# Second mixture of experts: TensorE waits for half of an expert's weights first, and for the rest at the second layer

## What is computed

```python
def _moe2_ref(x, w_skip, w_gate, w1, w2):
    do_compute = x @ w_skip > 0
    out = x.copy()
    xc = x[do_compute]
    e_idx = np.argmax(xc @ w_gate, axis=1)        # one expert for a token
    ...                                           # gate_w: its softmax weight
    for e in range(E):
        mask = e_idx == e
        h = np.maximum(xc[mask] @ w1[e], 0.0)     # w1[e]: 512 x 1024
        y[mask] = gate_w[mask, None] * (h @ w2[e])    # w2[e]: 1024 x 512
    out[do_compute] = xc + y
    return out
```

## Time and profile before

| | us |
|---|---|
| three timed runs | 730.63, 733.49, 738.72 |
| their median | 733.49 |
| the profiled execution, its own time | 731.53 |
| its span, first to last instruction | 729.7 |
| PE busy in the span | 652.2 (89%) |
| PE's mean granted clock, as a share of full speed | 0.952 |
| second mixture: first product of its experts | 526.3 |
| second mixture: last scatter issued | 719.6 |

### The profile page before, as it was taken

The page is one execution under the profiler, slowest core; times in us unless marked ns, Lnnn a source line. Parts: engine busy times, 40 slices in busy tenths (PEclk is TensorE's granted clock), DMA queues, the critical chain, the costliest instruction groups (busy, mean ns, idle before and its releaser), DMA issues.

```text
span 729.7 us, 13727 instructions
## 1 busy us (share of the span) xinstructions
PE 652.2 (89%) x4168; PEld 575.2 (79%) x4168; DVE 379.0 (52%) x761; ACT 292.8 (40%) x503; POOL 204.7 (28%) x227
## 2 busy tenths in 40 slices
PE   5697883799999999999999999999599979999793
PEld 4576763489999999999999999876487768777682
DVE  2676687535363545454453636403565476745721
ACT  2365662034352434443432435214155455645520
POOL 1538670220232405060413324030112222222220
PEclk9899997599999999999999999999799999999997
DMA  9999996126182727456371927167175587556221
GB/s 196 203 232 235 269 301 198 37 60 230 49 234 71 213 79 166 158 113 212 72 252 48 251 72 220 58 141 242 24 245 151 156 288 236 161 161 232 42 42 16
DMA packets 94866, 116.14 MB, mean 159 GB/s; under 512 B 55940, under 2 KB 56068, under 8 KB 94800
## 3 DMA queue, kind: packets, MB, share of 16 engines
q1 hardware_dynamic: 77264, 90.83, 41.9%
q0 software_dynamic: 10464, 23.81, 15.9%
q10 hardware_dynamic: 7072, 0.70, 0.7%
HBM read 100.01 MB, written 20.18 MB: 165 GB/s over the span
## 4 chain that ended last, share of the span: by engine, by line
PE 71%; SPq 8%; DMA 6%; DVE 6%; issue 5%; ACT 1%; POOL 1%; POOLq 0%; DVEq 0%; ACTq 0%
PE bank L788 20%; PE bank L794 20%; PE bank L893 15%; SPq L499 5%; DMA xg<-x_moe,ix_take 2%; PE bank L777 2%; SPq L514 2%; DMA out<-y_sb,ix_put 2%; PE bank L766 2%; PE bank L645 2%; PE bank L695 1%; PE bank L717 1%; PE bank L909 1%; DVE col_val L1580 1%; PE bank L678 1%
## 5 line engine op out<-in xcount | busy, mean ns | idle before, releaser
L1454 DVE TENSOR_TENSOR w_lo<-stage,w_hi x120 | 141.6, 1221 | 21.7 <-ACT w_hi L1018 19.5
L1018 ACT CAST w_hi<-stage x120 | 119.6, 1047 | 9.8 <-PEq L935 9.7
L788 PE MATMUL bank<-tok_hi,w_hi 128*128 128x416 f32 x256 | 91.3, 357 | 1.8 <-DVE tok_lo L1636 1.8
L794 PE MATMUL bank<-unit_hi,w_hi 128*128 128x416 f32 x256 | 92.5, 361 | 0.0
L788 PE MATMUL bank<-tok_hi,w_lo 128*128 128x416 f32 x256 | 90.5, 354 | 0.0
L794 PE MATMUL bank<-unit_lo,w_hi 128*128 128x416 f32 x256 | 90.2, 352 | 0.0
L794 PE MATMUL bank<-unit_hi,w_lo 128*128 128x416 f32 x256 | 89.6, 350 | 0.0
L1670 DVE SCALAR_TENSOR_TENSOR unit_lo<-bank,unit_hi 128x416 fp32r<-128x416 f32 x64 | 37.8, 591 | 98.2 <-ACT unit_hi L1104 98.2
L1104 ACT ACTIVATE unit_hi<-bank 128x416 fp32r<-128x416 f32 x64 | 33.2, 519 | 130.7 <-PE bank L788 130.7
L1304 POOL DMA_INDIRECT x_moe<-rows_out,ix_put x32 | 58.7, 1835 | 53.2 <-DVE rows_out L1659 45.9
L788 PE MATMUL bank<-tok_lo,w_hi 128*128 128x416 f32 x256 | 58.7, 350 | 0.0
(11 more groups left out here) (162 smaller groups left out, 1106.1 us busy)
## 6 DMA issues: line engine op xcount, KB each, us to landing
stage<-in_moe_w SPq DMA_DIRECT2D x128, 512.0 KB, 5.6
v_win<-in_v SPq DMA_DIRECT2D x24, 192.0 KB, 6.8
x_moe<-rows_out SPq DMA_DIRECT2D x12, 260.0 KB, 3.3
x_att<-x_sb POOLq DMA_DIRECT2D x12, 256.0 KB, 5.2
x_sb<-x_moe SPq DMA_DIRECT2D x12, 256.0 KB, 2.8
out<-x_moe SPq DMA_DIRECT2D x4, 768.0 KB, 8.6
late_raw<-in_v SPq DMA_DIRECT2D x6, 384.0 KB, 6.9
stage<-in_k SPq DMA_DIRECT2D x6, 256.0 KB, 6.7
```

The source lines that it names most:

```text
L788: last = eng.matmul(ps_unit[f % 2][:, 0:W], w, x, start=(i == 0), stop=(i == len(mine) - 1))
L794: last = eng.matmul(ps_out[chunk][:, 0:W], w[:, WC // 2 + f, chunk * P:(chunk + 1) * P], h[:, f % UNITS, :], start=(f == 0 and i == 0), st ...
L1018: eng.copy(piece(w_hi[n % SETS], j), stage[:, j, :]).then_inc(s_hi, 1)
L1454: eng.tensor_tensor(piece(w_lo[n % SETS], j), stage[:, j, :], piece(w_hi[n % SETS], j).bitcast(F32), ALU.subtract)\
```

## The change

PE's wait ahead of an expert's slots asks for `PIECES * n - 4` pieces, which are the expert's first four, the whole of `w1`. A new wait for all of the expert's pieces stands in each slot, between the first and the second layer. Nothing else differs.

```diff
                 for e in range(E):
                     n = m * E + e
                     hi, lo = w_hi[n % SETS], w_lo[n % SETS]
-                    eng.wait_ge(s_lo, PIECES * n)
+                    eng.wait_ge(s_lo, PIECES * n - PIECES // 2)
                     eng.reg_mov(done, 0)
                     with eng.While(lambda: eng.snap(done) < eng.snap(counts[e])):
@@
                         turn_h(0)
                         products(ps_h[1], up[1], T // 2, T).then_inc(S["h"], 1)
                         eng.wait_ge(S["hth"], sv * 2 + 1)
+                        eng.wait_ge(s_lo, PIECES * n)
                         eng.wait_ge(S["ye"], sv + 1)
                         products(ps_y, down, 0, T // 2)
```

## The result

The change makes the kernel faster by a little: 728.8 us against 733.9 us, medians of 20 runs each, with a ratio of 0.9929 and a 95% interval of 0.9906 to 0.9951. That is 5.2 us less (3.6 to 6.9). The ratio, and the 5.2 us worked out from it, leave out the few runs in a slower state. Forecast was a ratio of 730.0 / 733.5 = 0.995, 3.5 us less, which lies just outside the small end of that interval.

A forecast was written before the change was run, and what follows sets the result against it. POOL's serial DMA chain was taken to bind, 13.7 us per slot against PE's 13.0, hidden by two weight waits. `y_sb` at 714.3 instead of 717.84 gave 3.5 us less: 728.0 profiled, 730.0 us median; range 724.5 to 735.0.

The forecast's parts named there:

- the sum: Last slot's `y_sb` written at 714.3 instead of 717.84, 3.5 us less; profiled execution 728.0, median forecast 730.0 us.
- The end: Last slot: `y_sb` waits for scatter 12, landing at 714.06, and no longer for PE; written at 714.3.
- The waits and the clock: Before slots 5 and 12: PE starts 3.25 and 3.46 us earlier, and the low clock's 1.53 and 1.28 go too.
- The new wait at nothing: At the second layer, 14 times: passes with 3.4 us in hand, taken as no cost; upper end 1.4 us.
- DVE late in slot 5: PE waits 0.8 us for `ht_lo` in slot 5, leaving PE 4.0 us earlier after it.
- The gather at slot 9: At the turning of slot 9's rows, PE waits up to 3.7 us for POOL's gather; 4.0 us gain becomes 0.1.
- rival B: Earlier weight loads fall on more of POOL's gathers and scatters: 13 us on its chain, less 3.5, 743 us; chance 0.12.
- the mark of a wrong forecast: The forecast is wrong if POOL's steps between 589.99 and 646.42 shift by more than a microsecond.
- The size: Whole kernel: 3.5 us less, forecast 730.0 against 733.49 us, 0.5% less.
- Rival A: POOL keeps up and PE's whole gain comes through: 8.7 us, 724.8 us; chance 0.13.
- the argument against it: Against 743 us: an expert's 4 MB take some 13 us, a whole POOL round, and already meet one gather and scatter.

The follow-up runs named there:

- POOL relieved: The change with POOL's gather and scatter overlapped (ratio 0.9852), or with the last six experts' weight loads cut to an eighth (0.9867), both against the kernel before.
- slot 5 only: Kernel before, with the first wait asking for four pieces at the fourth expert only (slots 5 and 6): ratio 0.9963, 2.7 us less.
- Slot 12 alone: Kernel before, with the first wait asking for four pieces at the last expert only (slots 12 and 13): ratio 0.9958, 3.1 us less.
- the light loads: Last six experts' weight loads cut to 64 of each 512 columns: ratio 0.9986 on the kernel before, 0.9867 on the changed kernel.
- overlap, slot 5 only: Kernel before, with POOL's gather and scatter in flight together and four pieces asked for at the fourth expert only: ratio 0.9908, 6.8 us less.

## Why the prediction was right, and where not

The mechanism was right: both waits fall away, PE gains about 9.5 us of its own (9.7 and 8.8 with POOL relieved), and POOL's chain of one DMA at a time takes back a good part of it. The size agrees with the sum partly by luck, as said under *The end*. Point by point:

- *The waits and the clock.* Right, with 0.56 to 0.6 us left at each change of expert and a clock of 1.00.
- *The new wait at nothing.* Right, as far as one execution with nine of them tells.
- *DVE late in slot 5.* Of the forecast 0.8 us PE's row shows 0.2 in the changed kernel and 0.8 with slot 5 only.
- *The end.* Right: `y_sb` waits for scatter 12, forecast to land 714.06 - 526.27 = 187.8 us into the mixture, and it landed at 717.71 - 529.56 = 188.1. That these agree is luck in part. Scatter 3, ahead of the first removed wait, was issued 0.6 us later into the mixture than in the profile before. From there to scatter 7 POOL gained 1.6 us, where 0.1 was forecast. From scatter 7 to scatter 12 it lost 0.6 us (63.59 before, 64.15 after), where a gain of 0.64 was forecast; 1.0 of it is scatter 10, which took 5.9 us and not 4.9. Slot 12 alone gave 3.1 us, near the 3.4 that the sum leaves to it.
- *The gather at slot 9.* **This is the step that failed**: "PE waits up to 3.7 us there", and "4.0 us of gain have become 0.1". PE was held up along the way instead: 1.1 and 0.4 us at the second layers of slots 6 and 8, where `y_sb` was late because scatters 4 and 6 landed late. At slot 9's rows only 0.2 us were left, at slot 7's 0.3. The 0.8 us for slot 5's rows stand ahead of the first removed wait, and the second profile of the kernel before has them too. Of the 4.0 us, 1.1 were left at slot 9's rows, turned 118.0 us into the mixture and not 119.1 (2.1 in the second profile of the changed kernel, 116.9). I had kept the duration of each of POOL's DMAs as the trace before had it. But DVE's last five splits in slot 5 come earlier (from 76.6 us of the mixture on, before from 80.2), so the loads do, and by the GB/s above their burst moved from the gathers of slots 7 and 9 to the scatters of slots 4 and 6. With the light loads these long DMAs are gone. I had named that coupling in rival B and not in the sum. From the scatter at 589.99 to that at 646.42 POOL took 56.4 us before; the same scatters after stand at 593.91 and 648.77, 54.9 us. That is 1.6 less, more than the microsecond that I had set as the mark of a wrong forecast; in other profiles of the changed kernel and of slot 5 only it was 55.2 to 56.7, and 56.6 in the second profile of the kernel before, so the 1.6 is not a steady effect.
- *The size.* By the ratios slot 5's removal is worth 2.7 us (0.7 to 4.7) and not 0.1, which alone would cover the gap between 3.5 and 5.2. How POOL's chain lets that much through, and whether it is that much, is open: the profiles, one execution each, scatter by as much as is asked for.

Rival A's condition, that POOL keeps up, is what the light loads brought about, and its 8.7 us is near the 8.8 that they gave. Rival B's place was right and its sign not: one DMA of a pair got longer and the other shorter, and the four together stayed about the same, 23.1 us before and 22.4 after. That the loads fall on these DMAs already in the kernel before was the argument against it. Its 6.7 us for a slow gather stands in none of the rows; the earlier trace rows say 6.9, by which its 13 us would be 13.5.

## What to carry to other kernels

Before you count what a removed wait is worth, look for the serial chain on another engine that the wait had covered, and compare its time per round with the bound engine's: 13.7 against 13.0 us said that the gain would not come through whole. Do not keep that chain's durations fixed when the change moves the transfers that share its DMA engines, and look at every door by which it can hold you (here the gather, the output buffer, and the engine that fills it). Then remove the chain too: here the change was worth 5.2 us with it and 9.7 without it, each known to 2 or 3 us.

## What the runs showed of the hardware

- GpSimd's accumulating scatters move only the rows that a slot has, 0.01 to 0.26 MB here. With the light loads they land in 3.0 to 5.1 us: 3.0 and 3.2 for 0.01 MB, 4.7 to 5.1 for 0.26 MB. Under the weights' loads scatter 4, with 0.19 MB, took 8.3 us in the changed kernel, and 8.7 in the second profile of slot 5 only.
- A gather of 128 rows of 2 KB lands in 3.3 to 5.1 us with the light loads, and in up to 8.8 under them (overlap, slot 5 only).
- Eight further waits per slot, all of them passed already, changed the mixture of 14 slots by less than 0.1 us, in one execution.
- Transposes that nobody reads, 3.3 us of them, kept the granted clock at 1.00 behind a wait, where it had been 0.57 over 4 us.
